# Attention and two expert layers on one core: the x of a later stage loaded and prepared one attention step sooner, and four stash transfers put behind two others

## The reference, cut to what matters

```
scores = q @ k.T / 8 ; block-causal mask with blocks of 64 ; softmax ; @ v     # 4 x 8 heads, 576 rows, 64 wide
x = heads put side by side                                                     # (2304, 512)
out1 = sum over 4 experts e of  p[:, e] * (relu(x @ w1[e]) @ w2[e])             # 512 -> 1024 -> 512
h = out1 @ w_in ; solu = h * softmax(h) ; layer norm * g_ln ; @ w_out           # 512 -> 1024 -> 512
```

## Time and profile before

| | |
|---|---|
| median of three runs | 1160.36 us |
| the profiled execution | 1159.74 us |
| its span, first to last instruction | 1157.9 us |
| PE busy, of the span | 1138.7 us (98%) |
| DVE, ACT, POOL busy | 633.4, 428.5, 415.7 us |
| mean granted TensorE clock | 0.999 |
| bytes moved | 146.29 MB, 126 GB/s over the span |

### The profile page before, as it was taken

The page is one execution under the profiler, slowest core; times in us unless marked ns, Lnnn a source line. Parts: engine busy times, 40 slices in busy tenths (PEclk is TensorE's granted clock), DMA queues, the critical chain, the costliest instruction groups (busy, mean ns, idle before and its releaser), DMA issues.

```text
span 1157.9 us, 16760 instructions
## 1 busy us (share of the span) xinstructions
PE 1138.7 (98%) x6131; PEld 1020.9 (88%) x6131; DVE 633.4 (55%) x1139; ACT 428.5 (37%) x943; POOL 415.7 (36%) x403
## 2 busy tenths in 40 slices
PE   8999998989999999999999999999999999999998
PEld 7999988879999999999999999999998977888887
DVE  8999886454343424343433344353424468666765
ACT  7988885322223211122311113321112344434432
POOL 7998996654234100015300004500003463432330
PEclk9999999999999999999999999999999999999999
DMA  4766767983734222252405062503125100000001
GB/s 142 227 213 211 218 207 221 393 323 124 277 113 157 89 82 110 82 194 72 180 1 191 1 230 71 200 28 132 60 83 199 39 16 10 29 19 28 19 28 37
DMA packets 68342, 146.29 MB, mean 126 GB/s; under 512 B 6064, under 2 KB 34736, under 8 KB 68272
## 3 DMA queue, kind: packets, MB, share of 16 engines
q1 hardware_dynamic: 68272, 145.36, 36.2%
HBM read 114.60 MB, written 30.74 MB: 126 GB/s over the span
## 4 chain that ended last, share of the span: by engine, by line
PE 76%; POOL 1%; DVE 1%; DMA 1%; ACT 0%; issue 0%; SPq 0%; ACTq 0%; POOLq 0%
PE s L1723 34%; PE outp L1584 19%; PE s L1584 11%; PE ring L1584 10%; PE ring L1854 1%; DMA xr<-x_stash 1%; PE s L1797 1%; POOL x_late L761 0%; DMA x_stash<-x_tmp 0%; POOL yop_l L863 0%; DVE yop_l L1432 0%; ACT y_t L1108 0%; DVE acc L1378 0%; POOL x_tmp L785 0%; DVE ex L1504 0%
## 5 line engine op out<-in xcount | busy, mean ns | idle before, releaser
L1723 PE MATMUL s<-xr,w1s 128*128 128x384 f32 x2016 | 360.8, 337 | 4.9 <-DVE u L1414 2.5
L1723 PEld LDWEIGHTS s<-xr,w1s 128*128 128x128 f32 x2016 | 351.9, 189 | 9.7 <-DVE u L1414 2.8
L1061 ACT ACTIVATE hid_h<-u 128x384 fp32r<-128x384 f32 x96 | 50.4, 525 | 371.9 <-DVE u L1409 346.7
L720 POOL TENSOR_TENSOR work<-work 128x256 f32<-128x256 f32 x20 | 15.9, 797 | 393.8 <-DMA work<-in_moe_w 267.9
L1364 DVE SCALAR_TENSOR_TENSOR hid_l<-s,hid_h 128x384 fp32r<-128x384 f32 x48 | 26.7, 557 | 125.7 <-ACT hid_h L1057 125.7
L1723 PE MATMUL s<-w1s,yop_h 128*128 128x512 f32 x252 | 85.7, 399 | 1.9 <-POOL yop_l L863 0.7
L1322 DVE TENSOR_TENSOR u<-s,m_b 128x384 f32<-128x384 f32 x24 | 13.4, 557 | 131.9 <-PE s L1723 131.9
L1057 ACT ACTIVATE hid_h<-s 128x384 fp32r<-128x384 f32 x48 | 23.6, 491 | 155.6 <-PE s L1584 155.6
L1584 PE MATMUL s<-k_h,qb 128*128 128x288 f32 (+8 forms) x320 | 75.9, 324 | 3.3 <-ACT pr L906 1.7
L906 ACT ACTIVATE pr<-s,neg_max 128x576 f32<-128x576 f32 (+2 forms) x144 | 75.5, 537 | 3.3 <-DVE neg_max L1206 3.0
L1584 PE MATMUL outp<-w_h,hid_h 128*128 128x512 f32 x192 | 75.5, 393 | 0.0
(11 more groups left out here) (172 smaller groups left out, 2446.2 us busy)
## 6 DMA issues: line engine op xcount, KB each, us to landing
xr<-x_stash SPq DMA_DIRECT2D x77, 768.0 KB, 6.4
r_sb<-r_scratch SPq DMA_DIRECT2D x16, 576.0 KB, 4.3
x_rows<-x_n SPq DMA_DIRECT2D x32, 288.0 KB, 4.6
work<-x_rows SPq DMA_DIRECT2D x24, 384.0 KB, 6.7
x_stash<-x_tmp SPq DMA_DIRECT2D x12, 768.0 KB, 3.8
work<-in_moe_w SPq DMA_DIRECT2D x32, 256.0 KB, 3.9
stage<-in_moe_w SPq DMA_DIRECT2D x32, 256.0 KB, 5.1
x_stash<-xr SPq DMA_DIRECT2D x7, 768.0 KB, 9.8
```

Of the source, the lines that this page charges most:

```text
L720: pool.tensor_tensor(s1, a21, a22, ALU.add).then_inc(w1_sums, 1)
L1061: act.activation(hid[slot][0][:, :], source, ACT.Relu).then_inc(hid_high, 1)
L1723: last = pe.matmul(target, x, y, start=start and i == 0, stop=stop and i == 2, skip_group_check=True)
```

## The change

1. `load_x` waits for the stored rows of its own half t alone, not of both, and always loads all four pieces. (0,0) is issued in SP's step 8 behind `spread_r(8)`, not at the head of step 9. (0,1) is issued whole in step 11 behind `spread_r(11)`; before, two pieces went there and two at the head of step 12.
2. POOL does the join of (0,0) in step 8, its sums in 9, its low parts in 10 and 11 (before 9, 10, 11 and 13). (0,1) stays in steps 12, 13 and 14.
3. ACT does the casts of (0,0) in steps 9 and 10 (before 10 and 11), the first one of (0,1) in the middle of step 13 (before at its end), and the last one in `nearly_late` of step 14 (before in `late`).
4. `stash_first` of pieces 3 to 6 goes behind `stash_round` (1,0,2) and (1,0,3) in SP's list.

```diff
-            def load_x(sg, t, parts=(0, 1)):
-                for i in range(2):
-                    sp.wait_ge(x_stored[i], 16 * min(PAIRS, DC * (sg + 2)))
+            def load_x(sg, t):
+                sp.wait_ge(x_stored[t], 16 * min(PAIRS, DC * (sg + 2)))
                 if sg == 0 and t == 0:
                     sp.wait_ge(w1_ready, 3 * HALF_F)
-                elif parts == (1,):
-                    sp.wait_ge(x_added, 2 * sg + t)
                 elif 2 * sg + t < 3:
                     sp.wait_ge(x_low, NR * (2 * sg + t - 1) + 2)
...
             for p in range(PAIRS):
-                if p == 9:
-                    load_x(0, 0)
-                if p == 12:
-                    load_x(0, 1, (0,))
                 if p + 2 < PAIRS:
                     load_k(p + 2)
                 store_r(p)
                 spread_r(p)
+                if p == 8:
+                    load_x(0, 0)
                 if p == 11:
-                    load_x(0, 1, (1,))
+                    load_x(0, 1)
...
             load2(w2[0, :, :], 3)
-            stash_first(range(3, NP))
             stash_round(1, 0, 2)
             stash_round(1, 0, 3)
+            stash_first(range(3, NP))
             load_x(2, 0)
...
+                if p == 8:
+                    x_join(0, 0)
                 if p == 9:
-                    x_join(0, 0)
-                if p == 10:
                     x_add(0, 0, 0)
                     x_add(0, 0, 1)
-                if p == 11:
+                if p == 10:
                     x_low_part(0, 0, 0)
                     x_low_part(0, 0, 1)
+                if p == 11:
+                    x_low_part(0, 0, 2)
+                    x_low_part(0, 0, 3)
                 if p == 12:
                     x_join(0, 1)
                 if p == 13:
-                    x_low_part(0, 0, 2)
-                    x_low_part(0, 0, 3)
                     x_add(0, 1, 0)
                     x_add(0, 1, 1)
...
-                if p in (10, 11):
-                    x_cast(0, 0, p - 10)
-                if p == 14:
-                    x_cast(0, 1, 1)
+                if p in (9, 10):
+                    x_cast(0, 0, p - 9)
+                if p in (13, 14):
+                    x_cast(0, 1, p - 13)
 
             def nearly_late(p):
-                if p == 11:
+                if p == 10:
                     x_cast(0, 0, 2)
                 if p == 14:
                     x_cast(0, 1, 2)
+                    x_cast(0, 1, 3)
...
-                if p == 11:
+                if p == 10:
                     x_cast(0, 0, 3)
-                if p in (13, 14):
-                    x_cast(0, 1, 3 * (p - 13))
```

More of the change, by code:

```diff
@@ L544, in load_x @@
                     sp.wait_ge(x_added, 2 * sg + t)
-                for z in parts:
-                    rows = x_bottom if z else x_top
+                for z, rows in enumerate((x_top, x_bottom)):
                     for h in range(2):
```

## The result

The changed kernel takes 1163.44 us (8 runs, 1162.23 to 1165.37) against 1160.09 of the kernel before beside it (8 runs). The ratio is 1.003, with an interval of 1.0019 to 1.0041: slower by 3.4 us, where 1158.9 was forecast and nothing above 1161.6 was in the range. The profiled execution took 1163.21; before it was 1159.74.

What follows compares the result with a forecast made beforehand. TensorE has 98% of the span, with POOL, stash and operand transfer the chain before m2 of unit 4. That product starts 2.3 us sooner, 1.0 with the clock's fall; taken 1.5 off 1160.36 gives 1158.9, range 1155.8 to 1161.6.

Steps and rivals of the forecast that it cites:

- The load and join in step 9: Attention step 9: x lands about 114.2, POOL joins until 118.4, ACT's cast waits 2.8 us; cost 2.9 us, paid once.
- somewhat likelier than not: Step 9: PE's idle of some 2.5 us makes the clock fall, costing about 1.3 us (0 to 1.7).
- Of the excess ... take 2.5 as gone: Attention steps 10 to 13: of 2.84 us excess over steps without x work, 2.5 vanish (bounds 0.5 and 2.84).
- the queue of SP is no longer held in step 12 ..., so r, k and v of pairs 9 and 12 are not late: Attention step 12: SP no longer waits for the low parts, so these loads come in time; supports the 2.5 us gain.
- 0.93 + 0.37 + 0.34 = 1.64 and 1.49 go: Step 14 to m1 of unit 0: PE's four idles vanish, 1.64 and 1.49 us (bounds 1.0 and 3.13 for both).
- -2.7 at unit 0: Start of m1 of unit 0: sum of the attention terms, 2.7 us sooner without the clock's fall, 1.4 with it.
- The issue comes 2.7 sooner with everything else: Units' first stretch: stash round (1,0,2) is issued 2.7 us sooner, at 216.7, and lands at 220.5.
- of the second part of the change practically nothing: Stash order: of 6.9 us at PE only 2.3 reach the end, practically none of it from the new order.
- 14.2 us from about 218.6: Units' first stretch: 5.9 MB at some 415 GB/s, so x of (2,0) has landed at 232.8.
- the queue runs dry while POOL makes the low part of round 2: Rival, chance 0.15: pieces push x of (2,0), its join starts at 235 as before, operand chain gives nothing, 1160.3 us.
- the slower case: Rival, chance 0.12: POOL stays behind, +2.1 us at unit 0, dry queue adds 0.75, together +2.8: 1163.2 us.
- The link to the end: Join of x (2,0) to m2 of unit 4: steps keep their durations, and behind unit 4 nothing changes.

Runs made afterwards that it cites:

- x (0,1) later: Changed kernel with the load of x (0,1) moved from behind the spread of r(11) to behind the load of k(14): 1162.08 us, ratio 1.0018 to the kernel before.
- divisions in unit 3: Changed kernel with the normalising of the expert shares on VectorE done in unit 3 instead of unit 2: 1164.88 us, ratio 1.0037 to the kernel before.
- the one without halves: all mended, but the four pieces of x joined only when all have landed: 1155.84 us, ratio 0.9969 to the kernel before.
- attention part alone: Changed kernel with the stash order of before, pieces 3 to 6 ahead of rounds (1,0,2) and (1,0,3): 1160.56 us, ratio 1.0005 to the kernel before.
- mended attention: all mended with the stash order of the kernel before: 1157.06 us, ratio 0.998 to the kernel before.
- all mended: Changed kernel, x (2,0) and two rounds ahead of pieces 5 and 6, x (0,1) loaded later, its last cast late, x loaded and joined by halves: 1153.89 us, ratio 0.995.
- stash order alone: Kernel before with only the four operand pieces moved behind rounds (1,0,2) and (1,0,3): 1162.74 us, ratio 1.0022.
- filler: Kernel before with pieces 3 and 4 left ahead of rounds (1,0,2) and (1,0,3), pieces 5 and 6 moved behind them: 1159.85 us, ratio 0.9993.

## Why the prediction was wrong

**The load and join in step 9: right.** The cast in ACT's step 9 was to wait 2.8 us for the join, and the join for the load.

```profile
114.99 0.60 ACT L912 ACTIVATE ptr_h<-ring 128x512 fp32r<-128x512 f32 x1 [0.20 <-PE ring L1589]
117.84 0.84 ACT L949 ACTIVATE xr<-work 128x768 fp32r<-128x768 f32 x1 [2.26 <-POOL work L755]
```

It waited 2.26 behind a join that started at 114.05 (forecast 114.2) and took 3.77, not 4.15. PE fell back by 2.15 to 2.3 where 2.7 to 2.9 were forecast. The clock did not fall there in the changed kernel. It did with x (0,1) later, where nothing of step 9 is edited, and in two more kernels with the same step 9, divisions in unit 3 and the one without halves (idles of 2.25, 2.01 and 2.15 us). In the changed kernel and with the attention part alone (1.93 and 2.07) it did not. Three of five traces agree with "somewhat likelier than not".

**"Of the excess ... take 2.5 as gone": wrong.** Steps 10 to 13 start at 124.17 and step 14 at 172.01 (PE's first transpose of each), 47.84 us, where 46.80 stood before and 44.3 were forecast. The step that failed is "the queue of SP is no longer held in step 12 ..., so r, k and v of pairs 9 and 12 are not late". I counted what the queue lost and not what was put into it: x (0,1), issued at 141.52, goes whole in front of v (12), issued at 144.95. POOL waited 2.12 us for that v, the query of pair 14 came late behind it, PE idled 1.46 at 160.13, and the clock stayed low for most of 160 to 164. With the load moved, the four steps take 43.4, less than the forecast, but from a step 10 that began 3.2 us later, so that part of this may be ground made up. In the two kernels with the load moved and no fall of the clock in step 9, mended attention and all mended, they take 45.7 and 44.9. So at least 1.1 to 1.9 of the 2.5 were there to be had; the rest is not shown.

**"0.93 + 0.37 + 0.34 = 1.64 and 1.49 go": partly.** The wait of 1.49 for the low part in front of m1(0) is gone. In its place stands 1.31 for the reciprocals of the last pair, at 184.76. From step 14 to m1(0) it is 13.87 us in place of 16.49, so 2.6 of the forecast 3.1 came. The sum is 2.15 for step 9, 1.04 for steps 10 to 13, less 2.6: -2.7 at unit 0 came out as +0.6.

**"The issue comes 2.7 sooner with everything else": wrong in its link too.** The gain at m1(0) is not handed on whole. The 1.49 us in it are a wait of PE alone, and the loads hang on the last pair's row sums. Mended attention has m1(0) 3.16 us sooner than before, the load of x (1,0) 2.00 (185.81 against 187.81), the issue of round (1,0,2) 2.46 (216.97 against 219.43) and the join 2.88 (232.49).

**The stash order: the main error.** Two statements failed. The first is "of the second part of the change practically nothing": alone it costs 2.5 us, which is 2.4 us at the join. The second is "14.2 us from about 218.6": this lets the transfers run on from the end of the round's issue at 415 GB/s, and asks only for their order and their sum. It leaves out the time in front of the issue. While SP waits for POOL, nothing behind the wait can be in the queue, and the pieces were what the queue moved in that time. The rival named this ("the queue runs dry while POOL makes the low part of round 2") and gave it no loss, and the slower case priced it at 0.75 us. With the stash order alone the stretch 218 to 222 ran at 195 in place of 426 GB/s: 4 x 231 = 0.92 MB not moved, or 2.2 us at 426, nearly the whole 2.4 of the join. The two errors make up the miss: between the forecast start of m2(4), 252.90 - 2.3 = 250.6, and the measured 256.38 lie 5.8 us, of which some 3.3 are the gain that did not come at m1(0) and 2.4 the dry queue; such starts scatter by about 1 us between kernels with the same attention part, so the first figure is rough.

**The link to the end: right.** From join to m2(4) it was 17.5 us before and 16.9 to 18.4 in the other kernels, whose joins lie between 227.80 and 240.51. From m2(4) to the end of the span it was 905.0 before and 904.9 to 905.9 in all: the start of m2(4) tells the time. The idle of PE that does not count was named rightly: filler took away its 2.53 us for nothing. That ACT's cast behind the same stash round also held POOL's low parts, and so the join, until 235.24, the prediction did not see. Of the things to look for, the 3 to 4 us of idle for the operand transfer came as 1.69 + 0.55 + 0.56, at 252 and not at 245. Its signs of being wrong came too: m1(0) later than 184.5 (185.88), and m2(4) outside 249.5 to 252.5 (256.38). The idle for VectorE near 232 that was to go is there, 1.99 us, but behind the four divisions.

**The slower rival** gave 1163.2, close to the 1163.44, but for another reason: POOL did not stay behind after step 9. Its number is not evidence for it. The price that it gave the dry queue, 0.75, was a third of the 2.4 measured.

## What to carry to other kernels

Transfers that stand in a queue in front of an issue that waits are its filler: to move them behind it saves no byte and turns the wait into idle bandwidth. Before moving a DMA, read from the windows at that wait whether the queue is full, and leave there just what the wait can hide; behind it, put first the transfer that the chain asks for. Here the same bytes in three orders gave 1155.7, 1160.2 and 1162.7 us. And a load moved forward on a queue is paid by all that it passes: write down what stood behind its new place.

## What the runs showed of the hardware

**Small operations of DVE beside POOL.** Four operations of 128x18 elements took 4.56 us in the changed kernel, most of it while POOL added two tiles of 128x768 (3.62 us for both), single ones up to 1769 ns. With the attention part alone they took 1.42: the first began beside an addition of 128x384 that ended at 226.68 and took 761 ns, the other three ran with POOL idle and took 182 to 186 ns each. The Trainium skill, "SBUF — State Buffer", section SBUF: two separate sides, says that DVE operations with two SBUF inputs and GpSimd operations that read SBUF take turns on a shared pair of ports, each for its whole instruction. The trace agrees: the longest of the four, 1769 ns, is near the 1810 of one low part, and the 761 ns one, begun at 225.96, ends within 0.1 us of POOL's addition.

**The clock.** Behind single idles of PE of 2.25 us (x (0,1) later, 121.62) and 1.99 (changed kernel, 231.57) the granted clock went to its lower level. Behind 1.93 (changed kernel, 119.95), 2.07 (attention part alone, 119.96) and 2.73 (mended attention, 231.20) it did not. At the place of the late v(12) it did behind 1.46 (changed kernel, 160.13) and not behind 1.73 (attention part alone, 160.53). So the length of one idle alone did not tell it in these traces.

**A store in an empty queue** (round (1,0,2), 0.79 MB, changed kernel) landed 3.6 us after its issue, and 10.9 with the queue full. That store lands some 5.7 us sooner (at 224.7 against 230.3) and the kernel is slower: the landing of one transfer is not what the chain pays.
